# Two attentions and a mixing stage on one core: whole-row transposes, masks of two heads side by side, and masks behind all scores of a unit

## The chip, the cores and the metric

One core of one Trainium2 chip runs the whole program. The metric is the device time of one launch in microseconds. The kernel before took 561.27 us, the median of three runs (560.54 to 561.74).

## What is computed

For each of 4 batches there are three stages, one after the other (S is 576 tokens, 8 heads of 64 columns, so 512 model columns):

```python
# first attention: heads 0-3 local, heads 4-7 strided, both causal, stride 32
scores = q @ k.T / 8
mask_local   = (rel >= 0) & (rel < 32)
mask_strided = (rel >= 0) & (key % 32 == query % 32)
x = softmax(where(mask, scores, -1e9)) @ v
# mixing
theta = x @ w_theta
u = x + w_tok_r @ (x * cos(theta)) + w_tok_i @ (x * sin(theta))
x2 = u + relu(u @ w_ch)
# second attention: 4 experts of 64 columns, causal, the best 2 of 4 per token, weighted
out = sum over e of gate[:, e] * softmax(where(causal, x2@wq[e] @ (x2@wk[e]).T / 8, -1e9)) @ (x2@wv[e]) @ wo[e]
```

## The kernel before, in words

All work of an engine stands in one hand-written order: PROLOGUE (first attention of batch 0 and the mixing up to the waves), three times BODY (the end of a batch together with the first attention of the next) and EPILOGUE (the end of the last batch). Each engine walks the same list of steps and emits its part; waits between engines are semaphores with counted values. PSUM holds places taken in turn: two `wide` tiles of 1024 columns, two `turned` of 512 and two `acc` of 512.

The first attention handles a pair of heads at a time (`p` 0 to 3; 0 and 1 are local, 2 and 3 strided). Its steps on TensorE:

- **prep** (L1253) transposes the four whole 128-token tiles of q and of k, loaded by L604 into `raw_q` and `raw_k`.
- **tail** (L1264) transposes the last 64 tokens of q and of k, which L607 loads into rows 0 to 63 of the last tile of each. These are two transposes of 64 rows; VectorE copies the result into `qt` and `kt` (L966, L967).
- **scores** (L1275) first writes the mask of each of the two heads with a bf16 matmul (L1285): `copies` repeats a pattern of 32 rows (local) or 64 rows (strided) over the partitions, so both matmuls use the same first 32 or 64 rows. For local heads two small matmuls with `never` follow (L1295), and then the scores are added in 64-row, 32- or 54-column tiles, head 0 in the lower and head 1 in the upper half of the rows (L1305). VectorE takes the row maxima (L978), ScalarE the exponentials into `tiled`.
- **turn** (L1346) transposes `tiled`, five column tiles for a local pair and six for a strided one, the last with only 64 rows; **values** (L1380) multiplies with v, VectorE normalises into `x_tok`, and **back** (L1395) transposes `x_tok` in the same tiles, again with 64 rows in the last.

The second attention handles a pair of experts and a group of token tiles at a time: group 0 is token tiles 0, 1 and 2, group 1 is tile 3, group 2 (`LAST`) is the 64 tokens of tile 4 for both pairs together. **scores** (L1309) goes through the token tiles of the unit; for each it multiplies q and k in 64-row halves, one expert per half (L1326), and then adds the causal mask of the diagonal block with one bf16 matmul over all 128 rows for each expert (L1331). VectorE takes the maxima when the last mask of the unit is in (L982). **turn** (L1360) transposes the probabilities, **values** (L1419) multiplies them with v, key tile after key tile; key tile 4 has 64 rows.

Around the first attention's steps stand the projections, three matmuls for each product of split halves (L1227): **channel**, **qk**, **v**, **theta**, **wave**. `xu` (L861, L769) splits x after the last back of a batch for theta.

GpSimd makes the constants at the start; the semaphore `consts` is raised after the identity matrices, `masks` after the masks. `own()` is an increment of an otherwise unused semaphore on TensorE's queue.

SyncE issues the loads of q, k and v: those of pairs 0 and 1 when the z parts of the mixing are made (`load`), those of pair p + 2 when tail p (for v: values p) is done. In batch 0 ScalarE issues k for pairs 0 and 1.

Of the kernel before, what the change touches and what calls it, by code (L numbers as in the profile page):

```python
# [12 lines left out]
P = 128  # L13
# [292 lines left out]
def program(nc, q, k, v, w_theta, w_tok_r, w_tok_i, w_ch, w_gate, wq, wk, wv, wo, out):  # L306
    ctx = ExitStack()
    with ctx:
# [40 lines left out]
        with ExitStack() as zone:  # L349
            raw_q = sb("raw_q", [P, 2, NT, 2 * D], F32, zone)  # L350
            raw_k = sb("raw_k", [P, 2, NT, 2 * D], F32, zone)

            raw_v = sb("raw_v", [P, 2, L_T, DV], F32, zone)
            qt = sb("qt", [P, S], F32, zone)
            kt = sb("kt", [P, S], F32, zone)
            tiled = sb("tiled", [P, COLS, 2 * W], F32, zone)
            tiled_t = sb("tiled_t", [P, COLS * P], F32, zone)
            x_tok = sb("x_tok", [P, COLS, 2 * D], F32, zone)
# [18 lines left out]
        copies_l = sb("copies_l", [STRIDE, P], BF16)  # L377
        copies_s = sb("copies_s", [W, P], BF16)
        mask_l = sb("mask_l", [STRIDE, W], BF16)
        mask_s = sb("mask_s", [W, W], BF16)  # L380
# [219 lines left out]
        def load_half(eng, r, p, src, dst):  # L600
            slot = p % 2
            one = src[bass.ds(r, 1), 2 * p:2 * p + 2, :, :]
            for hh in range(2):
                eng.dma_start(dst[:, slot, 0:NT - 1, hh * D:(hh + 1) * D],  # L604
                              one[:, hh, 0:P * (NT - 1), :].rearrange("a (t p) d -> (a p) t d", p=P))\
                    .then_inc(s[f"qk_loaded{slot}"], 16)
            eng.dma_start(dst[0:TAIL, slot, NT - 1, :].rearrange("p (h d) -> p h d", h=2),  # L607
                          one[:, :, P * (NT - 1):S, :].rearrange("a h p d -> (a p) h d"))\
                .then_inc(s[f"qk_loaded{slot}"], 16)
# [87 lines left out]
        def _(pool):  # L697
# [27 lines left out]
            for t, n in ((copies_l, STRIDE), (copies_s, W)):  # L725
                of = t[:, :].rearrange("p (a n) -> p a n", n=n)
                after(g.affine_select(out=of, in_=of, compare_op=ALU.not_equal, fill=1.0, base=0,
                                      pattern=[[0, P // n], [-1, n]], channel_multiplier=1))
            rows = mask_s[:, 0:SQ].rearrange("p (c j) -> p c j", j=R_N)
            after(g.affine_select(out=rows, in_=rows, compare_op=ALU.is_ge, fill=MASKED, base=0,  # L730
                                  pattern=[[-R_N, R_T], [-1, R_N]], channel_multiplier=1))
            after(g.affine_select(out=mask_l[:, 0:STRIDE], in_=mask_l[:, 0:STRIDE], compare_op=ALU.is_ge, fill=MASKED,
                                  base=-1, pattern=[[1, STRIDE]], channel_multiplier=-1))
            after(g.affine_select(out=mask_l[:, STRIDE:W], in_=mask_l[:, STRIDE:W], compare_op=ALU.is_ge, fill=MASKED,
# [215 lines left out]
        def _(dve):  # L950
            v_ = nc.vector
            dve.wait_ge(s["consts"], 1)

            def emit(c, step, uses, note, r):
# [8 lines left out]
                if kind == "tail":  # L963
# [3 lines left out]
                    v_.tensor_copy(*turned_qk(kt, tail[:, P:P + TAIL], step[2], NB))\  # L967
# [249 lines left out]
        def _(pe):  # L1217
# [14 lines left out]
            def emit(c, step, uses, note, r):  # L1232
# [31 lines left out]
                elif kind == "tail":  # L1264
# [4 lines left out]
                    own()  # L1269
                    for n, raw in enumerate((raw_q, raw_k)):  # L1270
                        ins = nc.tensor.transpose(turned[slot][:, n * P:n * P + TAIL],
                                                  raw[0:TAIL, p % 2, NT - 1, :], ident[0:TAIL, 0:TAIL])
                    ins.then_inc(full["turned"][slot], 1)
                    note["prep"] = note["prep"] + [("turned", uses[0])]
                elif kind == "scores" and step[1] == "s1":  # L1275
# [4 lines left out]
                    if r == 0 and p == 0:  # L1280
                        pe.wait_ge(s["masks"], 1)

                    copies, mask = (copies_l, mask_l) if local(p) else (copies_s, mask_s)
                    for hh in range(2):
                        mm(wide[slot][:, hh * 512:hh * 512 + cols * W], copies[:, :],  # L1285
                           mask[:, :].unsqueeze(1).broadcast_to([part, cols, W]), start=True, stop=True,
                           skip_group_check=True)
# [21 lines left out]
                elif kind == "scores":  # L1309
# [8 lines left out]
                    for m, at0, _ in GROUPS[step[2]]:  # L1318
                        _, t0, rows = TOK[m]
                        n = t0 + rows  # L1320
                        for a0, a1 in [(0, min(512, n))] + ([(512, n)] if n > 512 else []):

                            for k, pair in enumerate(pairs_of(step[2], pr)):
                                for hh, slot in enumerate(slots):
                                    hd = slice(hh * HD, (hh + 1) * HD)
                                    mm(wide[slot][k * rows:(k + 1) * rows, at0 + a0:at0 + a1],  # L1326
                                       q3[hd, pair, t0:t0 + rows], k3[hd, pair, a0:a1], start=True, stop=True)
# [7 lines left out]
                elif kind == "turn":  # L1335
                    if step[1] == "s1":
                        part, nt, _, cols = tiles(step[2])
                        for n, (ca, cb) in enumerate(((0, 3), (3, cols))):
# [5 lines left out]
                            for t in range(ca, cb):  # L1344
                                k = min(P, part * nt - t * P)
                                ins = nc.tensor.transpose(turned[slot][:, (t - ca) * P:(t - ca) * P + k],  # L1346
                                                          tiled[0:k, t, :], ident[0:k, 0:k])
# [38 lines left out]
                elif kind == "back":  # L1386
                    p = step[2]
                    part, nt = tiles(p)[0:2]
                    for place, u, _ in note[("values", p)]:
                        pe.wait_ge(read[place][u[0]], u[1])  # L1390
                    for n, (ca, cb) in enumerate(parts(p)):
                        slot = free("turned", n)
                        for t in range(ca, cb):
                            k = min(P, part * nt - t * P)
                            ins = nc.tensor.transpose(turned[slot][:, (t - ca) * P:(t - ca) * P + k], x_tok[0:k, t, :],  # L1395
                                                      ident[0:k, 0:k])
                        ins.then_inc(full["turned"][slot], 1)
                elif kind == "values":
# [11 lines left out]
                    for k, pair in enumerate(pairs_of(step[2], pr)):  # L1410
                        for m, _, to0 in GROUPS[step[2]]:
                            _, t0, rows = TOK[m]
                            for j in range(m + 1):
                                n = TOK[j][2]
                                x = to0 + j * P + k * rows
                                for hh in range(2):
# [4 lines left out]
                                             start=j == 0, stop=j == m)  # L1421
# [154 lines left out]
```

## Time and profile before

| | |
|---|---|
| Median of the runs | 561.27 us |
| The profiled execution | 561.68 us, its span 559.9 us |
| TensorE | 538.1 us busy (96%), weight loads 455.5 us (81%) |
| VectorE | 320.1 us (57%) |
| ScalarE | 236.9 us (42%) |
| GpSimd | 109.5 us (20%) |
| Mean granted clock of TensorE | 0.994 of full |

The shares are of the span. A matmul's busy time overlaps that of the next, so distances between starts say more than durations. An fp32 matmul has two records in the trace. PEld is the weight load that belongs to a matmul.

### The profile page before, as it was taken

To read this page: it belongs to the slowest core of one execution; us is meant where nothing else is said; L and a number is where in the kernel's file an instruction comes from. 1 tells how busy PE (TensorE), PEld (TensorE's weight loads), DVE (VectorE), ACT (ScalarE), POOL (GpSimd) and SP (SyncE) were. 2 spreads that over 40 slices of the span, in tenths; PEclk is the share of its full clock that TensorE was granted. 3 is DMA by queue.
4 is the path that set the end of the run, shared out by engine and by line. 5 is a ranking of instruction groups with operands and counts; after the bars stand their busy time and mean duration, and the time that the engine had idled before them with its cause. 6 is when DMAs were issued, how large, how long until landed. Compare 5 with 4: busy or idle time off the path is not lost.

```text
span 559.9 us, 13648 instructions
## 1 busy us (share of the span) xinstructions
PE 538.1 (96%) x5593; PEld 455.5 (81%) x5593; DVE 320.1 (57%) x795; ACT 236.9 (42%) x599; POOL 109.5 (20%) x123
## 2 busy tenths in 40 slices
PE   7889999999999999999999999999999999999986
PEld 5566899988866799998876799998876689998764
DVE  0346948356888823255878831454779851343783
ACT  3462745444533551343542570255433571111452
POOL 4331440000231071000221152000213134000210
PEclk9899999999999999999999999999999999999999
DMA  9871217621000116411000013531000010000002
GB/s 214 177 174 26 52 39 189 136 61 28 2 2 2 37 49 125 88 45 45 2 2 2 19 67 75 96 83 31 21 1 0 20 67 1 1 2 1 1 1 85
DMA packets 79997, 28.97 MB, mean 52 GB/s; under 512 B 75200, under 2 KB 75200, under 8 KB 79936
## 3 DMA queue, kind: packets, MB, share of 16 engines
q1 hardware_dynamic: 74592, 25.88, 19.9%
q10 hardware_dynamic: 5344, 2.23, 1.9%
q8 instruction: 45, 0.74, 0.6%
q14 instruction: 16, 0.13, 0.1%
HBM read 23.37 MB, written 4.72 MB: 50 GB/s over the span
## 4 chain that ended last, share of the span: by engine, by line
PE 80%; DVE 7%; SPq 5%; ACT 2%; issue 2%; DMA 1%; POOL 1%; POOLq 0%; DVEq 0%; ACTq 0%
PE acc L1227 41%; PE wide L1227 16%; PE wide L1326 4%; PE turned L1419 3%; PE turned L1360 2%; SPq L604 2%; PE turned L1461 2%; DVE nmax L982 2%; PE turned L1346 2%; PE turned L1395 2%; PE wide L1380 2%; PE wide L1305 2%; PE turned L1260 1%; DMA raw_v<-in_v 1%; SPq L607 1%
## 5 line engine op out<-in xcount | busy, mean ns | idle before, releaser
L769 POOL TENSOR_TENSOR xu_lo<-xt,xu_hi 128x576 fp32r<-128x576 f32 x15 | 21.0, 1411 | 207.3 <-ACT xu_hi L861 207.3
L759 POOL TENSOR_TENSOR probs<-probs,weight 128x128 f32<-128x128 f32 (+4 forms) x36 | 26.9, 767 | 156.9 <-DVE weight L1036 156.9
L839 ACT ACTIVATE probs<-wide,nmax 128x128 f32<-128x128 f32 (+4 forms) x72 | 39.2, 554 | 36.0 <-DVE nmax L982 35.8
L834 ACT ACTIVATE tiled<-wide,nmax 128x64 f32<-128x64 f32 x176 | 39.2, 330 | 24.0 <-DVE nmax L978 20.2
L1227 PE MATMUL wide<-w_tok_hi,z_hi 128*128 128x288 f32 x216 | 47.5, 301 | 0.0
L1227 PE MATMUL wide<-w_tok_lo,z_hi 128*128 128x288 f32 x216 | 46.3, 295 | 0.0
L1227 PE MATMUL wide<-w_tok_hi,z_lo 128*128 128x288 f32 x216 | 46.3, 295 | 0.0
L850 ACT ACTIVATE pt<-turned 128x384 f32<-128x384 f32 (+1 forms) x32 | 16.5, 516 | 56.5 <-PE turned L1360 56.5
L1227 PE MATMUL acc<-xu_hi,w_ch_hi 128*128 128x288 f32 x128 | 39.3, 307 | 1.0 <-DVE xu_lo L1125 0.9
L1227 PE MATMUL acc<-x_hi,w_qk_hi 128*128 128x288 f32 x128 | 39.7, 310 | 0.0
L982 DVE TENSOR_REDUCE nmax<-wide 128x1 f32<-128x128 f32 (+4 forms) x72 | 33.9, 512 | 8.2 <-PE wide L1331 8.1
L776 POOL TENSOR_TENSOR z_lo<-absf,z_hi 128x512 fp32r<-128x512 f32 x20 | 26.3, 1313 | 59.2 <-ACT z_hi L898 59.2
L1227 PE MATMUL acc<-x_hi,w_qk_lo 128*128 128x288 f32 x128 | 37.7, 295 | 0.0
L1227 PE MATMUL acc<-xu_hi,w_ch_lo 128*128 128x288 f32 x128 | 37.7, 295 | 0.0
L1227 PE MATMUL acc<-xu_lo,w_ch_hi 128*128 128x288 f32 x128 | 37.7, 294 | 0.0
L1227 PE MATMUL acc<-x_lo,w_qk_hi 128*128 128x288 f32 x128 | 37.7, 294 | 0.0
L1227 PE MATMUL acc<-w_theta_hi,xu_hi 128*128 128x512 f32 (+1 forms) x80 | 34.6, 432 | 0.8 <-POOL xu_lo L769 0.5
L1227 PEld LDWEIGHTS wide<-w_tok_hi,z_hi 128*128 128x128 f32 x216 | 34.5, 189 | 0.8
L1227 PEld LDWEIGHTS wide<-w_tok_lo,z_hi 128*128 128x128 f32 x216 | 34.7, 189 | 0.0
L1227 PEld LDWEIGHTS wide<-w_tok_hi,z_lo 128*128 128x128 f32 x216 | 34.7, 188 | 0.0
L1360 PE MATMUL turned<-ident,probs 128*128 128x128 f32 (+1 forms) x200 | 29.8, 277 | 3.7 <-DVE probs L1029 1.3
L1089 DVE TENSOR_TENSOR absf<-turned,absf 128x512 f32<-128x512 f32 (+1 forms) x20 | 13.7, 684 | 33.9 <-PE turned L1461 33.9
(210 smaller groups left out, 1368.4 us busy)
## 6 DMA issues: line engine op xcount, KB each, us to landing
raw_q<-in_q SPq DMA_DIRECT2D x32, 128.0 KB, 2.4
out<-o_sb SPq DMA_DIRECT2D x16, 256.0 KB, 2.0
raw_k<-in_k SPq DMA_DIRECT2D x28, 128.0 KB, 2.5
raw_v<-in_v SPq DMA_DIRECT2D x14, 144.0 KB
raw_v<-in_v SPq DMA_DIRECT2D x14, 136.0 KB
raw_v<-in_v SPq DMA_DIRECT2D x32, 49.5 KB
raw_r<-in_moe_w_tok_r SPq DMA_DIRECT2D x1, 1152.0 KB, 6.3
stage<-in_moe_w_theta ACTq DMA_DIRECT2D x2, 512.0 KB, 7.4
```

The costliest lines, as they stand in the source:

```text
L759: ins = g.tensor_tensor(pr, pr, weight[:, j:j + 1].broadcast_to([P, n]), ALU.mult)
L769: g.tensor_tensor(xu[1][:, p, :], xt[:, p, :], xu[0][:, p, :].bitcast(F32), ALU.subtract)\
L776: g.tensor_tensor(z[1][:, chunk, :], src[:, m, :], z[0][:, chunk, :].bitcast(F32), ALU.subtract).then_inc(s["zl"], 1)
L834: e = a.activation(tiled[:, t, hh * W:(hh + 1) * W], wide[slot][:, at0:at0 + W], ACT.Exp, bias=nmax[:, hh, t:t + 1])
L839: e = a.activation(probs[:, hh, to0:to0 + n], wide[slot][:, at0:at0 + n], ACT.Exp, bias=nmax[:, hh, j:j + 1], accum_out=sums[:, hh, j:j + 1])
L850: ins = a.activation(dst, src, ACT.Copy)
L982: ins = v_.tensor_reduce(nmax[:, hh, j:j + 1], wide[u[0]][:, at0:at0 + TOK[m][1] + TOK[m][2]], AX.X, ALU.max, negate=True)
L1089: v_.tensor_tensor(absf[0:rows, m, :], x, absf[0:rows, m, :], ALU.mult).then_inc(s["zc"], 1)
L1227: ins = mm(place, lhs[x], rhs[y](cols), start=first and n == 0, stop=last and n == 2)
L1326: mm(wide[slot][k * rows:(k + 1) * rows, at0 + a0:at0 + a1], q3[hd, pair, t0:t0 + rows], k3[hd, pair, a0:a1], start=True, stop=True)
L1360: ins = nc.tensor.transpose(turned[slot][0:k, x:x + P], probs[:, hh, at0:at0 + k], ident[:, :])
L1419: ins = mm(turned[slot][hh * HD:(hh + 1) * HD, to:to + rows], v3[0:n, j, e * HD:(e + 1) * HD], pt[0:n, hh, x:x + rows], start=j == 0, stop ...
```

## The change

1. *Tail.* k's last 64 tokens are loaded into rows 64 to 127 of the last tile of `raw_q`, under q's; `raw_k` loses its last tile. One 128 x 128 transpose replaces the two of 64 rows, and `own()` goes from this step.
2. *Turn and back of the first attention.* The last transpose takes all 128 rows of its tile too. Nothing more of it is read than before.
3. *Masks of the first attention.* `copies` and `mask` are held twice, in rows 0 to 63 and 64 to 127 (for local heads rows 32 to 63 of each are zeros), so head 0 takes the first and head 1 the second half. VectorE makes the second halves with four copies at the start, for which it waits for GpSimd's masks; TensorE waits for the four copies.
4. *Scores of the second attention.* The masks of all token tiles of a unit follow behind all its scores. For this only the first matmul into a bank has the start flag. Only group 0 has more than one token tile.
5. *Values of the last token tile.* The second pair takes key tile 4 first, so that the two 64-row blocks are neighbours.

```diff
-            raw_k = sb("raw_k", [P, 2, NT, 2 * D], F32, zone)
+            raw_k = sb("raw_k", [P, 2, NT - 1, 2 * D], F32, zone)
...
-        copies_l = sb("copies_l", [STRIDE, P], BF16)
-        copies_s = sb("copies_s", [W, P], BF16)
-        mask_l = sb("mask_l", [STRIDE, W], BF16)
-        mask_s = sb("mask_s", [W, W], BF16)
+        copies_l = sb("copies_l", [P, P], BF16)
+        copies_s = sb("copies_s", [P, P], BF16)
+        mask_l = sb("mask_l", [P, W], BF16)
+        mask_s = sb("mask_s", [P, W], BF16)
...
-            eng.dma_start(dst[0:TAIL, slot, NT - 1, :].rearrange("p (h d) -> p h d", h=2),
+            rows = slice(0, TAIL) if dst is raw_q else slice(TAIL, P)
+            eng.dma_start(raw_q[rows, slot, NT - 1, :].rearrange("p (h d) -> p h d", h=2),
...
-            dve.wait_ge(s["consts"], 1)
+            dve.wait_ge(s["masks"], 1)
+            for t in (copies_l, copies_s, mask_l, mask_s):
+                v_.tensor_copy(t[W:P, :], t[0:W, :]).then_inc(s["masks"], 1)
...
-                    v_.tensor_copy(*turned_qk(kt, tail[:, P:P + TAIL], step[2], NB))\
+                    v_.tensor_copy(*turned_qk(kt, tail[:, TAIL:P], step[2], NB))\
...
-                    own()
-                    for n, raw in enumerate((raw_q, raw_k)):
-                        ins = nc.tensor.transpose(turned[slot][:, n * P:n * P + TAIL],
-                                                  raw[0:TAIL, p % 2, NT - 1, :], ident[0:TAIL, 0:TAIL])
-                    ins.then_inc(full["turned"][slot], 1)
+                    nc.tensor.transpose(turned[slot][:, 0:P], raw_q[:, p % 2, NT - 1, :], ident[:, :])\
+                        .then_inc(full["turned"][slot], 1)
...
-                        pe.wait_ge(s["masks"], 1)
+                        pe.wait_ge(s["masks"], 1 + 4)
...
-                        mm(wide[slot][:, hh * 512:hh * 512 + cols * W], copies[:, :],
-                           mask[:, :].unsqueeze(1).broadcast_to([part, cols, W]), start=True, stop=True,
+                        of = slice(hh * W, (hh + 1) * W)
+                        mm(wide[slot][:, hh * 512:hh * 512 + cols * W], copies[of, :],
+                           mask[of, :].unsqueeze(1).broadcast_to([W, cols, W]), start=True, stop=True,
...
-                                       q3[hd, pair, t0:t0 + rows], k3[hd, pair, a0:a1], start=True, stop=True)
+                                       q3[hd, pair, t0:t0 + rows], k3[hd, pair, a0:a1],
+                                       start=(at0 + a0) % 512 == 0, stop=True, skip_group_check=True)
+
+                    for m, at0, _ in GROUPS[step[2]]:
+                        _, t0, rows = TOK[m]
+                        n = t0 + rows
...
-                                k = min(P, part * nt - t * P)
-                                ins = nc.tensor.transpose(turned[slot][:, (t - ca) * P:(t - ca) * P + k],
-                                                          tiled[0:k, t, :], ident[0:k, 0:k])
+
+                                ins = nc.tensor.transpose(turned[slot][:, (t - ca) * P:(t - ca + 1) * P],
+                                                          tiled[:, t, :], ident[:, :])
...
-                            k = min(P, part * nt - t * P)
-                            ins = nc.tensor.transpose(turned[slot][:, (t - ca) * P:(t - ca) * P + k], x_tok[0:k, t, :],
-                                                      ident[0:k, 0:k])
+                            ins = nc.tensor.transpose(turned[slot][:, (t - ca) * P:(t - ca + 1) * P], x_tok[:, t, :],
+                                                      ident[:, :])
...
-                            for j in range(m + 1):
+
+                            order = [*range(m + 1)] if k == 0 else [m, *range(m)]
+                            for j in order:
...
-                                             start=j == 0, stop=j == m)
+                                             start=j == order[0], stop=j == order[-1])
```

## Rows read from the trace of the kernel before

**Rows 1.** The page's first line: busy us, share of the span, instructions.
```profile
PE 538.1 (96%) x5593; PEld 455.5 (81%) x5593; DVE 320.1 (57%) x795; ACT 236.9 (42%) x599; POOL 109.5 (20%) x123
```

**Rows 2.** Busy time by stretches: length, engines, granted clock, DMA share, GB/s.
```profile
0.00:38.00 38.00, 30.61 (x501) 21.58 (x504) 10.45 (x29) 18.44 (x56) 16.46 (x35) 0.96 0.95 206
...
99.00:144.00 45.00, 44.20 (x709) 39.95 (x708) 24.48 (x67) 21.63 (x66) 2.80 (x2) 1.00 0.31 66
...
158.00:178.00 20.00, 19.45 (x146) 13.89 (x145) 17.66 (x41) 8.00 (x24) 4.21 (x5) 1.00 0.00 1
```

**Rows 3.** The chain of waits in the prologue: start, us, what.
```profile
31.29 6.48 DMA raw_v<-in_v
```

**Rows 4.** TensorE's timeline at tail 0 of batch 1: start, us, what.
```profile
103.35 0.29 PE L1227 MATMUL acc<-xu_hi,w_ch_lo 128*128 128x288 f32 x1
...
103.57 0.27 PE L1271 MATMUL turned<-ident,raw_q 64*128 64x64 f32 x1
...
104.07 0.29 PE L1227 MATMUL acc<-xu_lo,w_ch_hi 128*128 128x288 f32 x1
...
103.57 0.13 PEld L1271 LDWEIGHTS turned<-ident,raw_q 64*128 64x128 f32 x1 [0.16 <-issue]
```

**Rows 5.** TensorE's timeline at the first prep of batch 1.
```profile
98.87 0.60 PE L1260 MATMUL turned<-ident,raw_q 128*128 128x128 f32 x4
...
99.87 0.29 PE L1227 MATMUL acc<-xu_lo,w_ch_hi 128*128 128x288 f32 x1
```

**Rows 6.** TensorE's timeline at tail 2 and behind it.
```profile
123.02 0.27 PE L1271 MATMUL turned<-ident,raw_q 64*128 64x64 f32 x1
...
123.51 0.28 PE L1227 MATMUL acc<-w_vg_lo,x_hi 128*128 128x260 f32 x1
```

**Rows 7.** TensorE's timeline before and behind back 1.
```profile
134.59 0.29 PE L1227 MATMUL acc<-x_hi,w_qk_lo 128*128 128x288 f32 x1
...
135.70 0.29 PE L1227 MATMUL acc<-x_lo,w_qk_hi 128*128 128x288 f32 x1
```

**Rows 8.** TensorE's timeline from turn 0 to the masks of pair 1.
```profile
116.20 0.80 PE L1346 MATMUL turned<-ident,tiled 128*128 128x128 f32 x5
...
116.93 0.44 PE L1285 MATMUL wide<-mask_l,copies_l 32*128 32x320 bf16 x2
...
117.08 0.29 PE L1285 MATMUL wide<-mask_l,copies_l 32*128 32x320 bf16 x1
```

**Rows 9.** TensorE's timeline in the second attention's first unit, some rows from narrow windows.
```profile
145.25 0.29 PE L1331 MATMUL wide<-mask_c,ident_b 128*128 128x128 bf16 x2
...
145.32 0.22 PE L1331 MATMUL wide<-mask_c,ident_b 128*128 128x128 bf16 x1
...
145.47 0.70 PE L1326 MATMUL wide<-k,q 64*128 64x256 f32 x4
...
145.79 0.38 PE L1326 MATMUL wide<-k,q 64*128 64x256 f32 x2
...
146.10 0.28 PE L1331 MATMUL wide<-mask_c,ident_b 128*128 128x128 bf16 x2
```

**Rows 10.** TensorE's timeline in the last token tile's values, from narrow windows.
```profile
192.41 1.37 PE L1419 MATMUL turned<-pt,v 128*64 128x64 f32 x26
...
192.94 0.84 PE L1419 MATMUL turned<-pt,v 128*64 128x64 f32 x18
193.00 0.78 PE L1419 MATMUL turned<-pt,v 128*64 128x64 f32 x16
```

**Rows 11.** The timeline at the start, GpSimd and VectorE.
```profile
4.35 0.24 POOL L739 TENSOR_SCALAR_AFFINE_SELECT mask_s<-mask_s 64x54 bf16<-64x54 bf16 x1
...
7.92 0.23 DVE L966 TENSOR_SCALAR qt<-turned 128x64 f32<-128x64 f32 x1 [7.92 <-PE turned L1271]
```

**Rows 12.** Timelines of VectorE, and of SyncE's DMA issues.
```profile
158.16 1.09 DVE L982 TENSOR_REDUCE nmax<-wide 128x1 f32<-128x128 f32 x3 [1.19 <-PE wide L1331]
...
93.04 0.63 SPq L607 DMA_DIRECT2D raw_k<-in_k  x1
```

More of the change, by code:

```diff
@@ L725, in _ @@
             for t, n in ((copies_l, STRIDE), (copies_s, W)):
-                of = t[:, :].rearrange("p (a n) -> p a n", n=n)
+                of = t[0:n, :].rearrange("p (a n) -> p a n", n=n)
                 after(g.affine_select(out=of, in_=of, compare_op=ALU.not_equal, fill=1.0, base=0,
                                       pattern=[[0, P // n], [-1, n]], channel_multiplier=1))
-            rows = mask_s[:, 0:SQ].rearrange("p (c j) -> p c j", j=R_N)
+            rows = mask_s[0:W, 0:SQ].rearrange("p (c j) -> p c j", j=R_N)
             after(g.affine_select(out=rows, in_=rows, compare_op=ALU.is_ge, fill=MASKED, base=0,
                                   pattern=[[-R_N, R_T], [-1, R_N]], channel_multiplier=1))
-            after(g.affine_select(out=mask_l[:, 0:STRIDE], in_=mask_l[:, 0:STRIDE], compare_op=ALU.is_ge, fill=MASKED,
+            after(g.affine_select(out=mask_l[0:STRIDE, 0:STRIDE], in_=mask_l[0:STRIDE, 0:STRIDE], compare_op=ALU.is_ge, fill=MASKED,
                                   base=-1, pattern=[[1, STRIDE]], channel_multiplier=-1))
-            after(g.affine_select(out=mask_l[:, STRIDE:W], in_=mask_l[:, STRIDE:W], compare_op=ALU.is_ge, fill=MASKED,
+            after(g.affine_select(out=mask_l[0:STRIDE, STRIDE:W], in_=mask_l[0:STRIDE, STRIDE:W], compare_op=ALU.is_ge, fill=MASKED,
                                   base=0, pattern=[[-1, STRIDE]], channel_multiplier=1))
@@ L1336, in emit @@
                     if step[1] == "s1":
-                        part, nt, _, cols = tiles(step[2])
-                        for n, (ca, cb) in enumerate(((0, 3), (3, cols))):
+                        for n, (ca, cb) in enumerate(parts(step[2])):
                             slot = free("turned", n)
@@ L1387, in emit @@
                     p = step[2]
-                    part, nt = tiles(p)[0:2]
                     for place, u, _ in note[("values", p)]:
```

## The prediction, made before the change had run

> **What bounds the kernel now.** I read the page's shares first [rows 1]: TensorE works in 96% of the span, the next engine, VectorE, in 57%. The table by stretches [rows 2] says where that holds. From 0 to 38 us TensorE is busy for 30.6 us of 38 while the DMA engines are at 0.95: this part waits for transfers. In the first attention of a batch (99 to 144 us) TensorE is busy for 44.20 of 45.00 us at the full granted clock, and a microsecond that leaves its queue there is a microsecond less. From 158 to 178 us VectorE has 17.66 of 20 us, but TensorE gives it the start. The chain of waits [rows 3] confirms the first handover: a transfer that lands at 31.29 + 6.48 = 37.77 us ends the transfer-bound start. VectorE's timeline [rows 12] shows the second: its chain in the second attention starts at 158.16, after 1.19 us of waiting for TensorE's scores.
>
> So every edit is priced by what it does to the distance between starts on TensorE. Starts say more here than durations, which overlap. The steady distance between 288-column matmuls is 0.133 us.
>
> **The short tails of the transposes.** In [rows 4] the last 288-column matmul starts at 103.35, so the next should at 103.483. In its place stand the two 64-row transposes, the first one's weight load held back 0.16 us; the row at 104.07 is the second matmul behind them, the first that keeps the old distance to its successor. The two cost 104.07 - 0.133 - 103.483 = 0.454 us. A transpose over all 128 rows costs far less than either [rows 5]: eight from 98.87, the second matmul behind them at 99.87, (99.87 - 0.133 - 98.87) / 8 = 0.108 us each. Nothing is lost at either edge. So what costs is going from the whole array to 64 rows and back, about 0.10 us in and as much out, with weight loads that no longer hide.
>
> The Trainium skill ("TensorEngine Tiling (Array Packing)", Key Properties) says that a change of tiling mode drains TensorE. The 0.16 us hold and the late second matmul of [rows 4] agree with it; by a rule that only counted columns the edit would be worth nothing, 128 columns being moved before and after.
>
> - *Tails of q and k*, four a batch. Tails 0 and 1 stand between whole-array matmuls: 0.454 - 0.108 = 0.345 each. Tail 2 follows the values, which are row-tiled too [rows 6]: 123.51 - 0.120 - 123.02 = 0.37, and the step out of tiling remains (0.07 to 0.15), so 0.17. Tail 3 waits for VectorE's copy of the transposes before it and keeps that wait, which hides its step in; it still saves its second transpose and its step out, so between the two: 0.23. Together 1.09 us a batch. Load count, bytes and the release of the buffer are the same (the next q and k loads wait for this step before and after), only half the rows land on other partitions: nothing.
> - *Backs.* Back 1 [rows 7]: from 134.723 to 135.70 - 0.133 = 0.844 us for five transposes; new 5 x 0.108 = 0.54, gain 0.30. Back 2 has the same neighbours, 0.28. Back 0's second part ends under VectorE's copy, which sets tail 3: nothing. Back 3 is followed by row-tiled scores: the step in moves, 0.04. Together 0.62.
> - *Turns.* They are followed by row-tiled masks or scores, so the step in is only moved from the last transpose to them. 116.20 to 116.93 [rows 8] becomes 5 x 0.108 + 0.10 = 0.64, gain 0.08 (a step from 64 to 32 rows goes with it); 0, 0 and 0.05 for the others. Together 0.13. The longer last transpose costs 0.054 each and is in these sums.
>
> **Masks of the first attention.** The two mask matmuls now start one after the other: 0.15 us apart for 320 columns [rows 8], which is what their columns take at the steady distance (0.133 x 320 / 288 = 0.148). Moved to different halves of the rows, and writing different halves of the wide tile as before, they may run together. The trace has no such pair in bf16 with many columns. The nearest row is the second attention's scores, fp32 in the same two halves: with 256 columns for each of two heads the four records take 0.63 us from the first start to the masks' [rows 9]. In sequence, at the 0.108 for 128 columns of [rows 5], they would need 0.86. So the heads run side by side. Bounds: 0 and 0.15 us a unit; I take 0.14, as the row with the same tiling does overlap. Four a batch: 0.56. The 32 zero rows added for the local heads add no column. The skill ("TensorE: Matmul & The Clock Gate", Part 3) has tiles in distinct row groups running together, up to 3.07 times for four; it agrees with the choice and no run here has shown it for bf16.
>
> **Second attention.** Only the unit of the first three token tiles changes. Its masks take 0.22 us a tile (145.25 to 145.47), the second tile's scores 0.63 [rows 9]. It looks as if the return to scores cost 0.2 us (256 columns for two heads side by side would take 0.43). But the second pair of the same tile is as late as the first: 145.47 to 145.79, 0.32 us for 0.216 of columns, and 0.31 more to the masks. So each pair pays about 0.10 for weight loads that don't hide; that is not the masks' price and stays. What goes is two of the three mask visits: 3 x 0.22 becomes 0.22 + 4 x 0.06 (two masks start 0.07 apart; their 128 columns alone would take 0.06). I take 0.20 a unit, bounds 0 and 0.6 (if the weight loads of the scores now hid as well). Two units a batch: 0.40. VectorE needs the whole unit anyway; the increments stay on the last mask of each head. In the first unit VectorE is still at the gates when the scores end, but TensorE goes on with projections that need nothing of it for 2 us.
>
> *Values of the last token tile* [rows 10]: pairs start 0.058 us apart; between the last whole-row pair at 192.41 and the second one behind the 64-row pairs of key tile 4, at 192.94, that block costs 192.94 - 0.058 - (192.41 + 0.058) = 0.41. There are two such blocks, with whole-row ones between them. Of that some 0.2 are the steps in and out, as for the tails. Side by side the blocks keep their pairs and lose one step in and out: 0.20 a batch.
>
> **Start.** VectorE waits for GpSimd's masks and makes four copies. GpSimd's last mask ends at 4.59 and four copies of about 0.23 us each, as its first instruction here takes for 64 columns, are done by 5.6 us; that first instruction comes at 7.92 [rows 11]. Cost 0 behind the wait for q and k; it would show only if the masks came 2 us later.
>
> **Sum.** A batch: 1.09 + 0.62 + 0.13 + 0.56 + 0.40 + 0.20 = 3.00 us. Three of them hold both attentions: 9.0. In the start everything before 37.8 us is worth nothing, as the DMA sets it; behind it come back 2 and turn 3, here both between whole-array transposes (0.28 each), and part of back 3 (0.09): 0.65. The last batch has the second attention alone: 2 x 0.20 + 0.20 = 0.6. Sum 10.25 us. The profiled execution took 561.68 us (span 559.9), 0.4 over the median: 551.4 for it, **551.2 us** against the median of 561.27.
>
> Is the gain kept? VectorE was idle 1.19 us before its chain at 158.16 [rows 12], more than the 0.2 that the unit itself wins, and what was won earlier moves VectorE's inputs too. The last q and k load that a batch begins with is issued at 93.04 and takes 0.63 us, and its first reader comes at 98.87 [rows 5, 12], so loads don't become the wait.
>
> **Rivals.**
> 1. *As summed*, 551.2, own range 549.6 to 552.9: chance 0.60.
> 2. *The bf16 masks don't overlap and the regrouped masks bring nothing*: 12 x 0.14 and 8 x 0.20 go, 10.25 - 3.3 = 7 us, 554.3. For it: no such bf16 pair in the trace. Chance 0.16.
> 3. *Scores also flow better without masks between them*: 8 x 0.4 more, 548.0. Against it the second pair inside a tile. Chance 0.08.
> 4. *Waits take half of it*: TensorE comes early to copies of VectorE and ScalarE. For it: tail 3 waits already, and in 158 to 178 us VectorE is full. Against it: it waits for TensorE before that. 10.25 / 2: 556.2. Chance 0.10.
> 5. *All of it is given back* at such waits, within 0.2%: 0.03.
> 6. *Slower*: the pauses belong to every first and last transpose of a short group and not to 64 rows. Then tails, turns and backs keep their edges and 24 turns and backs of the three batches are 0.054 us longer, 1.3 us: 562.6. It decides if a single whole-row transpose costs above 0.4 us; the eight of [rows 5], with 0.108 and no edge, speak against it. Chance 0.03.
>
> The range reaches from near rival 3 to the better half of rival 4: 548.5 to 555.5. Outside: most of 3, half of 4, 5 and 6, about 0.17. What differs by less than 0.2% can't be told from no change here. Faster 0.94, same 0.03, slower 0.03.
>
> **What would show it.** In the profile after: one 128 x 128 transpose per tail with the second matmul behind it at the old distance; no 64-row transposes in turns and backs; mask pairs starting together, under 0.05 us apart; six masks in one row of about 0.45 us; a batch of 126.6 us instead of 129.6. Wrong would be the forecast if single whole-row transposes show the same hold, or if TensorE's idle time between 99 and 178 us grows by over 1 us.

## The result, and the profile after

| | before | changed |
|---|---|---|
| Median of 4 runs | 561.22 us (560.54 to 561.74) | 547.76 us (546.18 to 549.85) |
| The profiled execution, its span | 561.68 us, 559.9 us | 546.84 us, 545.0 us |

The ratio is 0.9762, with a 95% interval from 0.9738 to 0.9786: 13.5 us faster. Forecast were 551.2 us and a range from 548.5 to 555.5. The direction was right, and the time fell 0.7 us below the range, where rival 3 (548.0 us) stood.

The page of the changed kernel, to be set beside [rows 1]:

```profile
PE 521.3 (96%) x5577; PEld 451.7 (83%) x5577; DVE 320.3 (59%) x799; ACT 236.7 (43%) x599; POOL 109.7 (20%) x123
```

TensorE has 16 records fewer, one for each tail (16 in the run, each now with one transpose for two), and 16.8 us less of busy time, nearly the 14.9 us by which the span is shorter. The other engines work about as long as before, and VectorE has four instructions more, the copies at the start. So the time went out of TensorE's own queue and, as a whole, did not come back as a wait. The stretch of the first attention in batch 1 shows the same: 44.28 us busy of 45.00 against 44.20 in [rows 2].

```profile
99.00:144.00 45.00, 44.28 (x724) 41.00 (x724) 26.77 (x77) 21.40 (x66) 4.21 (x3) 1.00 0.26 57
```

**Where in the run.** Each batch has one place that looks the same in all kernels here, the start of VectorE's addition of `wide` to `xt` in the mixing. Its timeline in the changed kernel, first and last of four:

```profile
96.90 0.76 DVE L1127 TENSOR_TENSOR xt<-wide,xt 128x576 f32<-128x576 f32 x1 [2.24 <-PE wide L1232]
...
474.63 0.76 DVE L1127 TENSOR_TENSOR xt<-wide,xt 128x576 f32<-128x576 f32 x1 [4.50 <-PE wide L1232]
```

Before, the same instructions started at 99.06 and 488.14. So a full batch took (488.14 - 99.06) / 3 = 129.69 us before and (474.63 - 96.90) / 3 = 125.91 now, 3.78 us less, where the sum had 3.00. Behind the last of them come 71.76 and 70.37 us: 1.39 less, where it had 0.6. Ahead of the first it is 2.16 us less (forecast 0.65), and most of that is not the edits' (last section). 3 x 3.78 + 1.39 + 2.16 = 14.89 us is the difference of the two spans.

The three batches are not alike before: 129.59, 129.52 and 129.97 us. In the third, VectorE starts one step late, the weighting of the probabilities behind a reciprocal. In the kernel before, batch 2 first, then the two instructions of batch 3:

```profile
307.30 0.55 DVE L1029 TENSOR_SCALAR probs<-probs,rec,gate 128x512 f32<-128x512 f32 x1
...
436.53 0.16 DVE L1020 RECIPROCAL rec<-den 128x1 f32<-128x1 f32 x1
437.15 0.55 DVE L1029 TENSOR_SCALAR probs<-probs,rec,gate 128x512 f32<-128x512 f32 x1 [0.46 <-DVE rec L1020]
```

From the reciprocal to that step it is 0.62 us, and 0.28 in batch 2. Since TensorE waits for the result there, the batch is about 0.35 us longer. All seven profiles without the four copies at the start of VectorE's queue have this late step in batch 3; none of the seven with them has it, and their three batches are equal within 0.05 us. So 0.35 us of the gain came with the copies and with no term of the forecast. Why is not known: no run has four other instructions in their place.

**The tail.** TensorE's timeline at tail 0 of batch 1, to be set beside [rows 4]:

```profile
101.18 0.30 PE L1232 MATMUL acc<-xu_hi,w_ch_lo 128*128 128x288 f32 x1
101.31 0.27 PE L1274 MATMUL turned<-ident,raw_q 128*128 128x128 f32 x1
101.34 0.38 PE L1232 MATMUL acc<-xu_hi,w_ch_hi 128*128 128x288 f32 x1
101.55 0.30 PE L1232 MATMUL acc<-xu_lo,w_ch_hi 128*128 128x288 f32 x1
```

By the rule that the forecast used: the second matmul behind the transpose starts at 101.55, so the tail costs 101.55 - 0.133 - (101.18 + 0.133) = 0.104 us (forecast 0.108, before 0.454). There is no held weight load.

**The chain of waits**, some pieces of batch 1 and one later: start, us, what.

```profile
101.47 0.11 PE turned L1274
101.58 1.59 PE acc L1232 x12
...
129.16 0.33 PE turned L1274
...
131.09 0.55 PE turned L1400 x5
131.64 1.58 PE acc L1232 x12
...
140.41 1.56 PE wide L1329 x12
141.97 0.44 PE wide L1339 x6
142.41 1.65 PE acc L1232 x12
...
186.47 1.61 PE turned L1426 x40
```

Read along the chain, tail 0 with the matmuls behind it gave 0.34 us, tail 1 0.35, tail 2 0.21, back 0 with tail 3 0.26, back 1 0.29, back 2 0.28. The forecast had 0.345, 0.345, 0.17, 0.23, 0.30 and 0.28. The values of the last token tile went from 1.75 to 1.61 (forecast 0.20 less). And each of the batch's two units of the second attention (scores and masks of one pair of experts) gave 0.52 us, where the forecast had 0.20. That is the miss. It is larger than these pieces show, since 0.09 us in each went back to the turns' and backs' edit (below).

**The start.** VectorE's copies lie where the forecast put them, 2.5 us ahead of the engine's next instruction (at 7.67), so no later step waits for them:

```profile
4.70 0.19 DVE L957 COPY copies_l<-copies_l 64x128 bf16<-64x128 bf16 x1 [4.70 <-POOLq L745]
...
4.99 0.17 DVE L957 COPY mask_s<-mask_s 64x64 bf16<-64x64 bf16 x1
```

### The profile page after: what moved, and what is told of

It reads as the page before. It is cut to its first block, busy times and chain, and to the rows that moved or that the text cites. A ratio compares the mean times of both kernels' runs of the same rounds, so it can differ in the third digit from the quotient of the medians.

```text
span 545.0 us, 13603 instructions
## 1 busy us (share of the span) xinstructions
PE 521.3 (96%) x5577; PEld 451.7 (83%) x5577; DVE 320.3 (59%) x799; ACT 236.7 (43%) x599; POOL 109.7 (20%) x123
## 4 chain that ended last, share of the span: by engine, by line
PE 79%; DVE 8%; SPq 5%; ACT 2%; issue 2%; DMA 1%; POOL 1%; POOLq 0%; DVEq 0%; ACTq 0%
PE acc L1232 41%; PE wide L1232 16%; PE wide L1329 4%; PE turned L1426 3%; PE turned L1367 2%; SPq L606 2%; PE turned L1468 2%; DVE nmax L987 2%; PE wide L1387 2%; PE wide L1308 2%; PE turned L1265 2%; PE turned L1400 1%; PE turned L1353 1%; DMA raw_v<-in_v 1%; SPq L610 1%
```

## The experiments

Each run of a kernel starts a little differently (last section), so the times of parts are read as us per batch, from the profile and by the two instructions above (the mean of three batches). The medians stand beside them. "Before" was measured anew with each group of runs. Theory A is that the masks between the scores cost what every change between 64-row and whole-row matmuls costs, a step out, a step in and a weight load that nothing hides, so that the unit gains its upper bound. Its rival B is the forecast: the lateness inside the scores belongs to the scores and stays, and the miss comes from elsewhere.

### One part alone

**Masks behind all scores, alone.** The kernel before with this edit:

```diff
-                                       q3[hd, pair, t0:t0 + rows], k3[hd, pair, a0:a1], start=True, stop=True)
+                                       q3[hd, pair, t0:t0 + rows], k3[hd, pair, a0:a1],
+                                       start=(at0 + a0) % 512 == 0, stop=True, skip_group_check=True)
+
+                    for m, at0, _ in GROUPS[step[2]]:
+                        _, t0, rows = TOK[m]
+                        n = t0 + rows
```

> The kernel before with the masks of the second attention behind all scores of a unit, nothing else. Theory A (every change between scores in 64-row halves and masks over all rows costs about 0.1 us in either direction and the first weight load behind it does not hide): a unit of three token tiles goes from 2.56 to 2.0 us, 8 units, 4.2 us less, ratio 0.9925. Theory B (the forecast: each pair of score matmuls pays its own weight load, only two mask visits are saved): 0.20 us a unit, 1.6 us less, ratio 0.997, and the scores of the second tile still take 0.63 us.

Measured: 556.02 us (554.65 to 557.43), ratio 0.993 (0.9907 to 0.9953). The chain of waits at the first unit:

```profile
142.79 1.47 PE wide L1326 x12
144.26 0.44 PE wide L1336 x6
144.70 1.65 PE acc L1227 x12
```

From the first score to the first matmul behind the masks it is 1.91 us; before it was 2.52. So 0.61 us a unit and not 0.20; a batch is 1.19 us shorter and the whole 4.4 us. The size is that of theory A.

**Tails alone** (the edits of `raw_k`, of its load, of the tail step and of L967).

> The kernel before with k's tail under q's and one transpose over all rows for both, nothing else. By the forecast 1.09 us a batch in three batches and nothing in the transfer-bound start: 3.3 us less, ratio 0.994. If the profile after is right about the start, 0.5 us more could come from there. Rival: the gain needs the neighbours' whole-row transposes too; then under 2 us.

Measured: 558.19 us (555.21 to 558.89), ratio 0.9956 (0.9935 to 0.9976). A batch is 1.21 us shorter, forecast 1.09.

**Turns and backs alone.**

The turns' half of the edit:

```diff
-                                k = min(P, part * nt - t * P)
-                                ins = nc.tensor.transpose(turned[slot][:, (t - ca) * P:(t - ca) * P + k],
-                                                          tiled[0:k, t, :], ident[0:k, 0:k])
+                                ins = nc.tensor.transpose(turned[slot][:, (t - ca) * P:(t - ca + 1) * P],
+                                                          tiled[:, t, :], ident[:, :])
```

> The kernel before with the last transposes of turn and back over all rows, nothing else. Forecast: 0.62 + 0.13 us a batch and 0.65 in the start, 2.9 us less, ratio 0.995. Rival (edges belong to every transpose group, not to 64 rows): 24 transposes longer by 0.054 us, 1.3 us more, ratio 1.002.

Measured: 558.17 us (556.1 to 560.58), ratio 0.9963 (0.9943 to 0.9983). A batch is 0.71 us shorter, forecast 0.75. The step into 64 rows moves to what follows: the first scores of a unit take 0.48 us in the chain instead of 0.39.

**Masks side by side alone.**

> The kernel before with the two masks of the first attention in different halves of the rows (four VectorE copies at the start, TensorE waits for them), nothing else. If bf16 matmuls in two halves run together: 0.13 to 0.16 us for each of 12 units in the batches, 1.7 us less, ratio 0.997, mask starts less than 0.05 us apart. If they do not: no difference, starts 0.15 us apart.

Measured: 559.01 us (556.5 to 560.95), ratio 0.9979 (0.9961 to 0.9998). A batch is 0.76 us shorter, forecast 0.56. The chain's rows for the four pairs of masks:

```profile
102.77 0.24 PE wide L1290 x2
...
113.95 0.14 PE wide L1290 x2
...
122.37 0.16 PE wide L1290 x2
...
134.64 0.16 PE wide L1290 x2
```

Before they were 0.37, 0.37, 0.33 and 0.33. Behind a whole-row matmul (the first) a pair takes 0.24, behind a turn that ends with 64 rows 0.14 to 0.16: there it needs no step into 64 rows any more, only its columns. The four together are 0.70 us shorter, and 0.13 comes back in the 44 records of the values at the end, 0.91 us instead of 0.78. The first two batches are 0.67 and 0.58 us shorter, near the forecast. The third is 1.04 shorter, as it lacks VectorE's late step.

**Order of the key tiles alone** (the edit of `order`), one run.

> The kernel before with only the order of the key tiles in the last token tile's values changed. The 40 records of a LAST group in the chain of waits go from 1.75 us to 1.61 (as the profile of the changed kernel has them) or 1.55 (as forecast), four groups, 0.6 to 0.8 us in all, which one run cannot tell from none.

Measured: 561.24 us. The piece of the chain is 1.61 us long, as in the changed kernel, so 0.14 us less. The three batches are 0.14, 0.17 and 0.30 us shorter, 0.20 in the mean; what more the third gave was not traced. The time itself tells nothing at this size.

Alone the parts give 1.19 + 1.21 + 0.71 + 0.76 + 0.20 = 4.07 us a batch, together 3.78. In the first two batches the gap is 0.15 us, and 0.10 of it is one step counted twice: the masks of pair 1 take 0.14 us behind the old turn and 0.24 behind the new one, which leaves them the step into 64 rows. In the third batch it is 0.56 us, and only a part of that is traced. The scores are no such case: the 0.09 us between their 1.56 in the changed kernel and 1.47 behind the old turn is already paid in the run with turns and backs alone.

### What is dear about masks between scores

**Two visits instead of three or one.** The kernel before; the scores of tiles 0 and 1, their masks, then tile 2 and its masks.

```diff
-                    for m, at0, _ in GROUPS[step[2]]:
+                    whole = GROUPS[step[2]]
+                    for some in ([whole[0:2], whole[2:3]] if len(whole) == 3 else [whole]):
```

> The kernel before with the scores of token tiles 0 and 1 first, then their masks, then tile 2 and its mask: two visits to the masks instead of three. Theory A (a price for each change of tiling, both ways) expects half of what the masks behind all scores gave, 0.3 of 0.61 us a unit, 8 units: 2.4 us less, ratio 0.9957. A rival (it is the distance between a score and the mask on the same columns that counts) expects nearly all of it for tile 0 and 1, which is two thirds: 3.3 us.

Measured: 557.94 us (556.08 to 560.4), ratio 0.9943 (0.9918 to 0.9968). The chain of waits:

```profile
144.66 0.82 PE wide L1328 x8
145.48 0.33 PE wide L1337 x4
145.81 0.84 PE wide L1328 x4
146.65 0.22 PE wide L1337 x2
```

The unit takes 2.21 us: 0.31 less for one visit less, 0.61 less for two. Each return from the masks to the scores costs the same. The median, 3.4 us under that of before, would fit the rival's 3.3; but a batch is 0.63 us shorter and the last one 0.56, 2.5 us in all, and the rest lies ahead of the first batch, where runs differ anyway. So theory A's 2.4 stands. The next run speaks against the rival too.

**Masks in the scores' own tiling.** The kernel before, the causal mask multiplied over 64 rows, with each expert in its own half as for the scores. It leaves out one half of each mask.

```diff
-                                ins = mm(wide[slot][k * rows:(k + 1) * rows, at0 + t0:at0 + n], ident_b[part, part],
-                                         mask_c[part, part], start=False, stop=True, skip_group_check=True)
+                                half = slice(hh * HD, (hh + 1) * HD)
+                                ins = mm(wide[slot][k * rows:(k + 1) * rows, at0 + t0:at0 + n],
+                                         ident_b[half, part], mask_c[half, part], start=False, stop=True,
+                                         skip_group_check=True)
```

> The kernel before with its order, masks after each token tile's scores, but each expert's mask matmul takes only the 64 rows of its own half of the array, as its scores do. It leaves out the other half of each mask (keys of that half of a diagonal block stay unmasked), so it is for its time alone. Groups 0 and 1 change, 16 units. Theory A: no change of tiling between scores and masks, so a unit of three tiles takes about 1.28 for scores, 0.2 to 0.3 at the edges and 3 x 0.06 for masks side by side, 1.8 us instead of 2.56, and a unit of one tile loses 0.1: 6 to 7 us less, ratio 0.988. Rival (a mask waits for the scores on the same columns, or the change from fp32 to bf16 costs): no difference.

Measured: 554.08 us (553.58 to 557.63), ratio 0.9884 (0.9832 to 0.9936). The chain of waits:

```profile
143.21 0.39 PE wide L1326 x4
143.59 0.06 PE wide L1332 x2
143.65 0.49 PE wide L1326 x4
144.14 0.06 PE wide L1332 x2
144.19 0.70 PE wide L1326 x4
144.89 0.06 PE wide L1332 x2
144.95 1.80 PE acc L1227 x12
```

A visit is down from 0.22 us to 0.06, and the scores of tile 1 take 0.49 instead of 0.63 although masks still stand between them. So bf16 beside fp32, and writing into columns just written, cost nothing to speak of. Some 0.06 us of the 0.16 that a visit lost are columns (128 of them at 0.133 us for 288), as the two masks now run side by side. The rest, and what the scores gained, is the change between 64 rows and the whole array. The last step out is not gone but moved, into the 12 projections behind, 1.80 us instead of 1.65.

### Undoing one part of the changed kernel

**Both masks from the lower half**, so that they run one after the other in 64 rows.

```diff
-                        of = slice(hh * W, (hh + 1) * W)
+                        of = slice(0, W)
```

> The changed kernel with both heads' masks of the first attention taken from rows 0 to 63. Then they can't run together: mask starts 0.15 us apart instead of together, 12 units in the batches, 1.6 to 2 us more than the changed kernel (ratio to before 0.980 where the changed kernel has 0.976). If running together was not what gained, no difference from the changed kernel.

Measured: 549.33 us (549.05 to 550.04), ratio 0.9785 (0.9754 to 0.9817), 1.64 us above the changed kernel of the same group of runs; a batch is 0.51 us longer. The pairs take 0.37, 0.37, 0.43 and 0.43 us instead of 0.24, 0.24, 0.27 and 0.27. Two bf16 masks in two halves do run side by side, worth 0.13 to 0.16 us a pair; the forecast took 0.14.

**The changed kernel once more**, as the measure for that.

> The changed kernel again, as the partner for the others of this call and for its start: if the warm-up matmuls behind the first values and the landing of v (2.16 us earlier for the start of the first batch in the profile after) belong to the change, they come again, 96.9 us; if they vary from execution to execution, as the four kernels with one part each already suggest (96.2 to 99.9 us), this one lies anywhere in that range. Ratio to before 0.976 to 0.978.

Measured: 547.69 us (546.81 to 548.12), ratio 0.9752 (0.9721 to 0.9784); a batch 125.91 us, as before.

**Masks between the scores again**, all else changed.

> The changed kernel with the masks of the second attention put back between the scores of the token tiles. Theory A (each return from whole-row masks to the 64-row scores costs a step, an unhidden weight load and a step out again): a unit is 0.52 to 0.61 us longer, eight units, 4.2 to 4.9 us more than the changed kernel, 552.2 us, 0.984 of the kernel before. Less if this part overlaps with the others and they were counted twice.

Measured: 551.86 us (550.42 to 554.49), ratio 0.9839 (0.9806 to 0.9872), 4.1 us above the changed kernel's 547.76 of another group of runs. The chain of waits:

```profile
139.44 0.48 PE wide L1329 x4
...
141.83 0.22 PE wide L1334 x2
```

2.60 us from 139.44 to the next piece at 142.04, against 2.00 in the changed kernel (140.41 to 142.41): 0.60 us a unit. A batch is 127.03 us, 1.12 longer, and the last one 1.21: 4.6 us in all, as expected.

**The held increment back ahead of the tails.** `own()` went together with the 64-row transposes, so the 0.345 us of a tail could have been the increment's.

> The changed kernel with the increment that stood ahead of the tails put back (16 in all). If a part of the 0.345 us that a tail lost belonged to the held increment and not to the 64-row transposes, at least 0.6 us comes back over 16 tails. By theory A (the whole of it is the entry into 64 rows and the step out) nothing comes back: the tail stays at 0.11 us, the 12 matmuls behind it at 1.59, and the time is that of the changed kernel within 0.3 us.

Measured: 548.78 us (547.79 to 549.99), ratio 0.977 (0.9749 to 0.979). Tails 0 to 2 are unchanged (0.11, 0.11 and 0.26 us in the chain, 1.60, 1.58 and 1.45 behind them). Tail 3, which waits for VectorE, is later by some 0.15 us: a batch is 126.05 us, 0.14 longer. Neither of the two expectations holds to the letter, since 3 x 0.14 = 0.4 us came back. The rest of the 1.0 us between the medians is not in the batches: in the profile this run's first batch came 2.76 us later, mostly by the clock (last section). What the lone tails lost belongs to the 64 rows.

### One step further

**Token weights on whole rows.** The start transposes the 64 last tokens' tiles of the token weights in nine groups, between whole-row transposes.

```diff
+            for t in (raw_r, raw_i):
+                v_.memset(t[TAIL:P, NT - 1, :], 0.0)
...
-                        ins = nc.tensor.transpose(place, src, ident[0:rows, 0:rows])
+                        ins = nc.tensor.transpose(place, src, ident[:, :])
```

> The changed kernel with the last 64 tokens' tiles of the token weights (nine groups at the start) transposed over all 128 rows, the unused 64 rows zeroed once by VectorE. By theory A each of these 64-row groups stands between whole-row ones and loses about 0.28 us: 2.0 to 2.5 us less than the changed kernel, 545.3 us, 0.972 of the kernel before. Rival: the start is set by the copies of ScalarE and VectorE and by the loads, so that less than 1 us comes.

Measured: 547.4 us (546.69 to 548.12), ratio 0.9744 (0.9727 to 0.9761); its interval overlaps the changed kernel's, so the medians show no difference. The profile does. In the mixing of batch 0 the piece of 12 matmuls behind a group of five transposes takes 1.59 us, and 1.78 in the run with the increment, whose start is otherwise alike; the period of such a round is 2.94 us against 3.22.

```profile
73.85 0.55 PE turned L1550 x5
74.39 1.59 PE wide L1234 x12
...
76.79 0.55 PE turned L1550 x5
```

0.28 us a group, as theory A has it, but for five of the nine groups: 1.4 us, where 2.0 to 2.5 were expected. From the second group of 44 records to the first batch it is 51.34 us instead of 52.73, the same 1.4. So the first four groups gave nothing that lasts; they stand in the part of the start where TensorE waits for others.

## Why the forecast was wrong: the masks behind all scores

The step that failed stands under "Second attention": "So each pair pays about 0.10 for weight loads that don't hide; that is not the masks' price and stays." It made the forecast 0.20 us a unit, inside bounds of 0 and 0.6. The upper bound came true: 0.61 us alone, and 0.60 when in the changed kernel the masks go between the scores again. (The changed kernel's own unit is only 0.52 shorter than before, since the whole-row transposes ahead of it leave it their step of 0.09.)

The observation was sound, the cause was not. Before, the two pairs of tile 1 took 0.32 and 0.31 us for 0.213 us of columns each [rows 9]. The two delays have two causes, and both are the masks'. The first pair stood right behind the return to 64 rows, with a weight load that nothing hid. The second pair's own columns took 0.213; the other 0.10 was the step out to the whole-row masks, the same that the forecast had itself priced at 0.10 for the tails, and that the distance to the next mask's start contains. Two equal numbers were read as one cause. The weight loads of the changed kernel, rows of the timeline, agree:

```profile
140.37 0.98 PEld L1329 LDWEIGHTS wide<-k,q 64*128 64x128 f32 x12 [0.20 <-issue]
141.90 0.34 PEld L1339 LDWEIGHTS wide<-mask_c,ident_b 128*128 128x128 bf16 x6 [0.55 <-issue]
```

The loads of the twelve score records run on ahead of the matmuls, and the engine of loads is idle only before the first of them (0.20 us) and before the first mask's (0.55), which starts with its matmul at 141.90. TensorE's own rows, some from narrow windows, are the proof:

```profile
140.40 1.57 PE L1329 MATMUL wide<-k,q 64*128 64x128 f32 x12
140.70 0.95 PE L1329 MATMUL wide<-k,q 64*128 64x256 f32 x6
141.13 0.84 PE L1329 MATMUL wide<-k,q 64*128 64x384 f32 x4
141.45 0.52 PE L1329 MATMUL wide<-k,q 64*128 64x384 f32 x2
141.90 0.51 PE L1339 MATMUL wide<-mask_c,ident_b 128*128 128x128 bf16 x6
```

Tile 1 (140.70 to 141.13) takes 0.43 us instead of 0.63, which is 256 columns for two heads side by side: both of its delays are gone. Tile 2 separates the two causes. It follows scores now and is still followed by masks, and its first pair is on time (0.32 us for 0.32 of columns) while its last is late (0.45). Before, both were late, 0.43 and 0.42:

```profile
146.32 0.59 PE L1326 MATMUL wide<-k,q 64*128 64x384 f32 x2
146.75 0.49 PE L1326 MATMUL wide<-k,q 64*128 64x384 f32 x2
147.17 0.28 PE L1331 MATMUL wide<-mask_c,ident_b 128*128 128x128 bf16 x2
```

If each pair paid for its own weight loads, the first pair of tile 2 would still be late. The experiments tell this from the rivals: price by the visit (0.31 and 0.61 us for one and two fewer), none left when the masks share the scores' tiling, back when the masks go between again. The Trainium skill ("TensorEngine Tiling (Array Packing)", Key Properties) says that switching the mode drains TensorE, which the forecast applied to the tails and not here, where both edges of each mask visit are such switches. The rows agree with the rule and give the price that it leaves open: 0.31 us for a visit saved, 0.11 of it in the mask pieces of the chain (3 x 0.22 against 0.44) and 0.20 in those of the scores.

**The terms of the sum**, us per batch:

| part | forecast | alone, measured | |
|---|---|---|---|
| tails | 1.09 | 1.21 | right; tails 0 and 1 to 0.01 |
| turns and backs | 0.62 + 0.13 | 0.71 | right |
| masks side by side | 0.56 | 0.76 | right; 0.63 in the first two batches, and VectorE's late step in the third is 0.12 of the mean |
| masks behind all scores | 0.40 | 1.19 | the step above |
| order of key tiles | 0.20 | 0.20 | right mechanism; its own piece gave 0.14 |
| all | 3.00 | 4.07, together 3.78 | |

Three batches gave 11.34 us where the forecast had 9.0. The last batch gave 1.39 where it had 0.6, since its two units were two of the eight that were undersized. With 0.61 in place of 0.20 a unit the sum would have been 10.25 + 8 x 0.41 = 13.5 us. That this is the measured difference is partly chance: the parts overlap by 0.29 us a batch and the start gave 0.5 us less, and against that stand terms that gave somewhat more and VectorE's late step. What the batches, the last batch and the start show is 11.34 + 1.39 + 0.12 = 12.85 us, with the 0.35 of that late step in it; the medians, whose runs spread over 1 to 4 us, lie 13.5 apart.

**The start** was overestimated: 0.12 us of 0.65. From the matmuls behind the last landing to those of the next pair's values (44 records each) it is 6.85 us in the changed kernel and 6.95 to 6.97 in two kernels with the old transposes and the same clock; from there to 96.90 both take 52.7. What the shorter transposes saved became idle time: between 42 and 60 us TensorE is busy for 16.92 us of 18 in the changed kernel and for 17.59 in the kernel with only the masks behind, at the full clock in both. The forecast's three terms there (back 2, turn 3 and a part of back 3) lie in a part that other engines pace.

**The gain was kept**, as forecast. In the batches TensorE's busy share between 99 and 144 us did not fall, and VectorE's chain still waits for TensorE's masks when it starts. But that wait is 0.56 us where it was 1.19 [rows 12]; about as much again and VectorE would take over there:

```profile
152.58 1.09 DVE L987 TENSOR_REDUCE nmax<-wide 128x1 f32<-128x128 f32 x3 [0.56 <-PE wide L1339]
```

**The rivals.** Rival 2 fell in both halves. Rival 3, the scores flowing better, had 0.08 and was the truth. Rivals 4 and 5, waits that take the gain, show in the start, with 0.5 us, and perhaps in the values that took 0.78 us at 139.09 before and take 0.87 at 134.84 now. Rival 6, edges of every short group, fell with the 0.104 us of the lone whole-row transpose. The range was built as if the bounds of the unit (0 and 0.6) were mostly a matter for a rival with 0.08; 8 x 0.4 = 3.2 us hung on one reading of two distances, and with a chance of 0.3 for the upper bound the range would have had to reach down to it.

## What to carry to other kernels

Count the changes between 64-row and whole-row matmuls on a TensorE that is the bound, not the columns: here 0.35 us more for a lone pair of 64-row transposes between whole-row work than for one whole-row transpose of the same data, and 0.31 us for each visit of whole-row masks among 64-row scores. Sort the work of a unit by tiling, or widen the odd tile, which here cost at most 0.054 us of columns for a transpose. When two distances are both too long by the same amount, ask of each what stands at its start and what at its end before one cause is given to both; and when an explanation makes a term three times smaller than its upper bound, give the upper bound a chance worth that doubt.

## What the runs showed of the hardware

- **A pair of 64-row bf16 masks inside 64-row work costs 0.06 us** for 128 columns each, and whole-row ones 0.22, with 0.14 us more in the scores behind them. In one tiling the two halves of the array run side by side in bf16 as in fp32 (0.24 against 0.37 us for 2 x 320 columns).
- **The clock behind the landing of the last load in the start** differs from run to run, whatever the edit. Stretch from 39 to 42 us in the profile of the changed kernel, of its repetition, and of the kernel with the tails alone; the column after the busy times is the granted clock:

```profile
39.00:42.00 3.00, 3.00 (x22) 2.42 (x20) 1.40 (x3) 0.71 (x2) 0.00 (x0) 1.00 0.00 0
```

```profile
39.00:42.00 3.00, 3.00 (x18) 2.17 (x16) 0.69 (x2) 0.71 (x2) 0.00 (x0) 0.72 0.00 0
```

```profile
39.00:42.00 3.00, 3.00 (x8) 2.37 (x9) 1.28 (x3) 0.00 (x0) 0.00 (x0) 0.50 0.00 0
```

  Full speed is 2.4 GHz and 0.50 is 1.2 GHz. TensorE had waited for `raw_v` before. At the lower level all of this stretch the way between the two groups of 44 records takes 9.57 to 9.81 us (four profiles) instead of 6.82 to 6.97 at full speed, almost 3 us. The kernel before had 0.59 there in its profile and 8.53 us: 1.57 of the 2.16 us that its first batch was longer are that, and 0.50 an earlier landing (37.32 against 37.82). This is why the parts were measured from batch to batch: the shared place of the first batch came anywhere between 95.94 and 99.89 us, mostly by this. What decides the clock there was not tried.
- **The held increment costs only where TensorE has to wait**: nothing at tails 0 to 2, some 0.15 us at tail 3.
- **VectorE's late step** in the third batch, 0.35 us, is there in seven profiles without the four copies at the start of its queue and in none of seven with them, 430 us after these have run. What causes it was not tried. To measure a part by its batches, look at each batch and not at the mean alone.
